# First stage of a fused mLSTM and MLP kernel: u spread by TensorE, decays by a product, weights split in quarters on GpSimd

## The chip, the cores and the metric

The kernel runs on 1 core of one Trainium2 chip. The metric is device time in microseconds (us). The engines are PE (TensorE), DVE (VectorE), ACT (ScalarE), POOL (GpSimd) and SP (SyncE, which only issues DMAs here).

## What is computed

An mLSTM recurrence over 4 batches x 8 heads x 768 steps with head size 40, and then two MLP layers over the 3072 tokens of 320 features. Cut from the reference:

```python
for t in range(S):
    m_new = np.maximum(f_gate[:, :, t] + m, i_gate[:, :, t])
    f_stab = np.exp(f_gate[:, :, t] + m - m_new)
    i_stab = np.exp(i_gate[:, :, t] - m_new)
    m = m_new
    C = f_stab[:, :, None, None] * C + i_stab[:, :, None, None] * np.einsum('bhd,bhe->bhde', vt, kt)
    n = f_stab[:, :, None] * n + i_stab[:, :, None] * kt
    h_tilde = np.einsum('bhde,bhe->bhd', C, qt)
    denom = np.maximum(np.abs(np.einsum('bhd,bhd->bh', n, qt)[:, :, None]), 1.0)
    y[:, :, t] = o * h_tilde / denom
...
h = x @ w_in                                   # 320 -> 2048
x = (np.maximum(h, 0) + alpha * np.minimum(h, 0)) @ w_out
h = np.maximum(np.maximum(x @ w1, x @ w2), x @ w3)   # 320 -> 768, three times
out = h @ w_out2
```

## The kernel before

The recurrence is computed in 24 chunks of 128 steps (8 heads at once): within a chunk as masked products, between chunks by a carried state. The chunks are grouped in 7 blocks (of 2, 3, 3, 4, 4, 4 and 4). While the first MLP layer of block b runs on PE, the chunks of block b+1 are computed between its matmuls; the second MLP layer comes last. So only the chunks 0 and 1 (block 0) stand ahead of all matmuls of the MLP. This is the first stage, and its order is `PLAN_FIRST`, written by hand; `block_plan` gives the order after it. Each engine goes through the same list of steps (`EVERY`) and takes out its own part, strictly in order; semaphores join them.

The stages of the first stage, with the lines of before:

- Gates (DVE, L864 to L875): a running maximum over 768 steps for the 32 rows (batch, head), then for each half of the sequence the decay, its sum within a chunk (`U`, by a scan of 128 steps for each chunk, L873) and `V`. `gates_done` counts the halves. The inputs of these instructions are all in SBUF. ACT makes `E` and `W` out of them (L725 to L730), PE transposes `V`, `E`, `W` (L521), and DVE copies the result into `tables` (L883).
- Mask and exponent of a chunk: `U` is stored to DRAM (L413), and each chunk's row is loaded again into all 128 partitions (`load_u`, L408, into `u_bcast`). POOL masks it ("prepare", L1098) and weighs the values with a table (L1091); ACT takes exp with a table as bias ("gate", L769). DVE multiplies the product of queries and keys (PE, L553) with it ("scores", L908).
- The state ("carry"): PE L561 and L568, DVE L920 to L930. Its last step on DVE, L930, adds the decayed state, which POOL makes (`state_decayed`, L1137) from a table of decays. That table is one row of `tables`, stored to DRAM (L439) and loaded into all partitions (L442).
- "values" (PE L583, DVE L940), "finish" (DVE L950 to L961) and "turn" (PE L602, ACT L759, DVE L967 and L968) end a chunk in `x_split`, which the MLP reads. Chunks from the third on also need "pack": the values split in three bf16 parts by ACT (L750, L753) and POOL (L1122, L1125), and the probabilities split by DVE (L912) and POOL (L1131).
- The weights of the first MLP layer are split into a high part (ACT `high_piece`, L707, L711, L712) and the rest (`low_piece`, L365, L369, L371) on DVE or POOL. `PIECES` lists the ten pieces: six of 128 x 1024 for w_in, four of 128 x 1280 for w_out. `ACT_PIECES`, `DVE_PIECES` and `POOL_PIECES` say after which step of the list an engine does which. PE's "hidden" (L627) and "project" (L641 to L646) of block 0 wait for them.

## Time and profile before

| | us |
|---|---|
| median of 3 runs | 793.49 (793.34 to 794.3) |
| the profiled execution | 794.83 |
| its span in the trace | 793.1 |
| PE busy | 745.3 (94%) |
| DVE busy | 477.2 (60%) |
| ACT busy | 310.1 (39%) |
| POOL busy | 184.1 (23%) |

The span is the time from the first to the last instruction in the trace; 1.7 us lie around it. Busy shares are means over the whole span; PE's first 71 us are far less filled than the rest.

### The profile page before, as it was taken

How to read it: one execution, taken by the hardware profiler on the slowest of the kernel's cores; microseconds unless marked ns; L12 is line 12 of the kernel's file. 1: busy time of each engine (PE TensorE's matmuls, PEld its weight loads, DVE VectorE, ACT ScalarE, POOL GpSimd, SP SyncE). 2: the span in 40 equal slices, each digit the busy share in tenths (PEclk: the TensorE clock that was granted, in tenths of full speed). 3: DMA queues.
4: the chain of work that ended last, by engine and by line, in shares of the span. 5: the costliest groups of instructions: out<-in, count | busy, mean ns of one | idle time of the engine just before them, and what ended most of it. 6: DMA issues, size and time to landing. Idle time of an engine off the chain costs nothing.

```text
span 793.1 us, 11547 instructions
## 1 busy us (share of the span) xinstructions
PE 745.3 (94%) x4410; PEld 656.1 (83%) x4410; DVE 477.2 (60%) x823; ACT 310.1 (39%) x648; POOL 184.1 (23%) x187
## 2 busy tenths in 40 slices
PE   2556999999999999999999999999999999999997
PEld 2545999999998888888888888888888888888886
DVE  6345888878978786888688754934242432434222
ACT  4354455455356444644554245431211212121211
POOL 4277533334524332434233200000000000000000
PEclk9757999999999999999999999999999999999999
DMA  7961232223223221231110053030110202000000
GB/s 203 259 215 61 78 102 72 101 75 105 69 81 105 88 79 58 87 105 61 42 54 1 1 182 120 1 110 4 36 39 0 74 1 74 0 34 1 34 0 34
DMA packets 40057, 56.37 MB, mean 71 GB/s; under 512 B 3457, under 2 KB 29058, under 8 KB 39618
## 3 DMA queue, kind: packets, MB, share of 16 engines
q1 hardware_dynamic: 39570, 54.57, 22.3%
q10 hardware_dynamic: 432, 1.06, 0.4%
q8 instruction: 35, 0.57, 0.3%
q14 instruction: 20, 0.16, 0.1%
HBM read 47.65 MB, written 7.96 MB: 70 GB/s over the span
## 4 chain that ended last, share of the span: by engine, by line
PE 83%; DVE 7%; POOL 3%; DMA 2%; SPq 2%; issue 1%; ACT 1%; ACTq 0%; DVEq 0%; POOLq 0%
PE bank L663 25%; PE bank L627 20%; PE bank L641 5%; PE bank L643 5%; PE bank L642 5%; PE bank L553 4%; PE bank L677 3%; PE bank L679 3%; PE bank L678 3%; PE bank L645 3%; PE bank L646 2%; PE bank L561 1%; PE bank L568 1%; POOL wproj L369 1%; PE bank L590 1%
## 5 line engine op out<-in xcount | busy, mean ns | idle before, releaser
L627 PE MATMUL bank<-x_split,w_hi 128*128 128x512 f32 (+2 forms) x560 | 170.7, 372 | 2.2 <-ACT x_split L759 2.2
L627 PE MATMUL bank<-x_split,w_lo 128*128 128x512 f32 (+2 forms) x336 | 121.9, 365 | 0.0
L627 PEld LDWEIGHTS bank<-x_split,w_hi 128*128 128x128 f32 x560 | 103.9, 191 | 16.2 <-ACT x_split L759 2.6
L795 ACT ACTIVATE g_full<-bank 128x512 f32<-128x512 f32 (+2 forms) x112 | 59.8, 534 | 143.7 <-PE bank L627 142.0
L993 DVE SCALAR_TENSOR_TENSOR g_full<-g_full,beta,bank 128x512 f32<-128x512 f32 (+2 forms) x112 | 74.7, 667 | 38.4 <-ACT g_full L795 37.5
L641 PE MATMUL bank<-g_hi,wproj 128*128 128x512 f32 (+2 forms) x224 | 84.9, 379 | 3.5 <-DVE g_lo L974 3.5
L1014 DVE TENSOR_TENSOR best<-bank,first_of_max 128x512 f32<-128x512 f32 x36 | 24.9, 692 | 103.9 <-PE bank L663 77.4
L804 ACT ACTIVATE g_hi<-g_full 128x512 fp32r<-128x512 f32 (+2 forms) x112 | 63.2, 564 | 61.4 <-DVE g_full L993 61.3
L974 DVE TENSOR_TENSOR g_lo<-g_full,g_hi 128x512 fp32r<-128x512 f32 (+2 forms) x112 | 70.3, 627 | 18.9 <-ACT g_hi L804 18.1
L643 PE MATMUL bank<-g_hi,wproj 128*128 128x512 f32 (+2 forms) x224 | 81.5, 364 | 0.0
L642 PE MATMUL bank<-g_lo,wproj 128*128 128x512 f32 (+2 forms) x224 | 81.4, 363 | 0.0
L834 ACT ACTIVATE g_hi<-best 128x512 fp32r<-128x512 f32 x36 | 22.8, 632 | 130.4 <-DVE best L1018 130.4
L663 PE MATMUL bank<-x_split_b,w_hi 128*128 128x512 f32 x270 | 71.5, 394 | 0.0
L1131 POOL TENSOR_TENSOR prob<-prob_rest 128x512 bf16<-128x512 f32 x44 | 49.1, 1117 | 93.8 <-DVE prob_rest L912 93.8
L627 PEld LDWEIGHTS bank<-x_split,w_lo 128*128 128x128 f32 x336 | 64.4, 192 | 7.4
L663 PE MATMUL bank<-x_split_a,w_hi 128*128 128x512 f32 x270 | 70.3, 390 | 0.0
L769 ACT ACTIVATE u_bcast<-u_bcast,tables 128x128 f32<-128x128 f32 x192 | 59.8, 390 | 9.1 <-POOL u_bcast L1098 9.1
L663 PEld LDWEIGHTS bank<-x_split_b,w_hi 128*128 128x128 f32 x270 | 50.0, 188 | 10.4
L663 PEld LDWEIGHTS bank<-x_split_a,w_hi 128*128 128x128 f32 x270 | 50.0, 188 | 9.5
L553 PE MATMUL bank<-q_t,k_t 120*128 120x128 f32 x384 | 51.3, 290 | 4.5 <-DVE inner L940 4.5
L553 PEld LDWEIGHTS bank<-q_t,k_t 120*128 120x128 f32 x384 | 50.3, 206 | 5.8 <-DVE inner L940 4.6
L641 PEld LDWEIGHTS bank<-g_hi,wproj 128*128 128x128 f32 x224 | 42.5, 190 | 9.0 <-issue 2.8
(115 smaller groups left out, 1399.6 us busy)
## 6 DMA issues: line engine op xcount, KB each, us to landing
u_bcast<-u_scratch SPq DMA_DIRECT2D x24, 512.0 KB, 4.4
kv<-in_kv SPq DMA_DIRECT2D x24, 324.0 KB, 3.0
out<-final SPq DMA_DIRECT2D x6, 640.0 KB, 3.8
q_t<-in_q_t SPq DMA_DIRECT2D x24, 120.0 KB
k_t<-in_k_t SPq DMA_DIRECT2D x48, 60.0 KB
wproj_raw<-in_w_out SPq DMA_DIRECT2D x4, 640.0 KB, 10.5
o_gate<-in_o_gate SPq DMA_DIRECT2D x4, 640.0 KB, 4.8
w_raw<-in_w_max SPq DMA_DIRECT2D x2, 1152.0 KB, 6.5
```

The costliest lines, as they stand in the source:

```text
L553: ins = pe.matmul(ps[:, k * L:(k + 1) * L], kt[0:KR, c, h, :], qt[0:KR, c, h // KH, :], start=True, stop=True)
L627: ins = pe.matmul(ps[:, 0:cols], w[:, a, f], xs[:, x, 0:cols], start=(m == 0), stop=(m == 7))
L641: pe.matmul(acc[a][:, 0:cols], wa, hi, start=(j == 0), stop=False)
L642: pe.matmul(acc[a][:, 0:cols], wa, lo, start=False, stop=False)
L643: pe.matmul(acc[a][:, 0:cols], wl, hi, start=False, stop=(j == J1 - 1))
L663: ins = pe.matmul(ps[:, :], w[:, a, cols], x2[b2 % 2][:, x, :], start=(k == 0), stop=(k == 7))
L769: ins = act.activation(ub[:, c, h, :], ub[:, c, h, :], ACT.Exp, bias=tables[:, 0, ch, h:h + 1])
L795: act.activation(gf[:, n % GF_SLOTS, 0:cols], hid[j % HID_BANKS][:, 0:cols], ACT.Relu, scale=-1.0).then_inc(neg_done, 1)
L804: act.activation(gh[:, n % G_SLOTS, 0:cols], gf[:, n % GF_SLOTS, 0:cols], ACT.Copy).then_inc(g_hi_done, 1)
L974: dve.tensor_tensor(gl[:, n % G_SLOTS, 0:cols], gf[:, n % GF_SLOTS, 0:cols], gh[:, n % G_SLOTS, 0:cols].bitcast(F32), ALU.subtract).then_i ...
L993: dve.scalar_tensor_tensor(out=g, in0=g, scalar=beta[:, j:j + 1], in1=hid[j % HID_BANKS][:, 0:cols], op0=ALU.mult, op1=ALU.add).then_inc(h ...
L1131: pool.tensor_tensor(prob_3[:, heads, :], prob_r[:, heads, :], high(prob_r[:, heads, :]), ALU.subtract).then_inc(prob_split, 1)
```

## The change

Only the first stage and the weight pieces change.

1. For the chunks 0 and 1 (`ON_PE` = 2) `u` is not stored and loaded again. PE spreads it: for each half of the heads 4 matmuls of bf16 that put the mask into a bank (`later`, MASKED where a key is later), and 4 f32 matmuls that add the head's row of `U` (`bcast`). POOL doesn't mask these chunks, and ACT reads the bank.
2. The table of decays is a product of PE with a matrix that has ones in its last row (`decays`), copied by DVE; the store and the load are gone.
3. The gates are computed in the spans of chunks 0 to 1 and 2 to 5 instead of two halves; `chain` 0, 1 and 2 stand at three places of the list. Chunk 0 has no "carry" product, since the state ahead of it is zero.
4. w_in is loaded and split in four quarters (12 pieces of 128 x 512); w_out stays in four. POOL does all rests, DVE none.
5. The clears of `k_t` are on DVE, one for each slot; `i_gate` is loaded by ACT's queue. On SP's queue `o_gate` of block 0 comes after chunk 0. The store and the load of `u` for chunk 2 are issued by ACT ("exps" 1), which waits for the store between the two.
6. The turn of chunk 0 stands ahead of the finish of chunk 1, and the exponents of chunk 2 ("gate" 2) behind both turns; the high parts of w_out's last two quarters stand on ACT among the first "hidden" steps.

```diff
-    steps = [("prepare", 0), ("prepare", 1), ("gate", 0, 0), ("gate", 0, 1), ("scores", 0), ("carry", 0),
-             ("gate", 1, 0), ("gate", 1, 1), ("values", 0), ("scores", 1), ("finish", 0, 0), ("finish", 0, 1),
-             ("prepare", 2), ("carry", 1), ("values", 1), ("gate", 2, 0), ("gate", 2, 1), ("pack", 2, 0),
-             ("finish", 1, 0), ("finish", 1, 1), ("pack", 2, 1), ("prepare", 3)]
-    return steps + [("turn", 0), ("turn", 1)]
+    return [("chain", 0), ("exps", 0), ("products", 0), ("turns", 0), ("bcast", 0), ("turns", 1), ("bcast", 1),
+            ("tables", 0), ("gate", 0, 0), ("gate", 0, 1), ("chain", 1), ("tables", 1), ("prepare", 0),
+            ("scores", 0), ("chain", 2), ("values", 0), ("carry", 0), ("gate", 1, 0), ("gate", 1, 1),
+            ("exps", 1), ("prepare", 1), ("products", 1), ("scores", 1), ("finish", 0, 0), ("finish", 0, 1),
+            ("turns", 2), ("tables", 2), ("decays",), ("carry", 1), ("values", 1), ("turn", 0), ("finish", 1, 0),
+            ("finish", 1, 1), ("turn", 1), ("prepare", 2), ("gate", 2, 0), ("gate", 2, 1),
+            ("pack", 2, 0), ("pack", 2, 1), ("prepare", 3)]
...
-
-PIECES = [("in", a, half) for half in range(2) for a in range(3)] + [("out", n, 0) for n in range(4)]
-ACT_PIECES = {("gate", 0, 1): (2, 3), ("gate", 1, 1): (3, 5), ("gate", 2, 1): (5, 6), ("pack", 2, 1): (6, 10)}
-DVE_PIECES = {("carry", 0): (2, 3)}
-POOL_PIECES = {("prepare", 2): (3, 5), ("prepare", 3): (5, 10)}
+TASKS = [(part, s[1]) for s in EVERY for part in parts_of(s)]
+
+IN_PARTS, OUT_PARTS = 4, 4
+
+
+def pieces():
+
+    order = [("in", a, 0) for a in range(3)]
+    for q in range(1, IN_PARTS):
+        order += [("in", a, q) for a in range(3)] + [("out", q - 1, 0)]
+    return order + [("out", OUT_PARTS - 1, 0)]
+
+
+PIECES = pieces()
+IN_END = [PIECES.index(("in", 2, q)) + 1 for q in range(IN_PARTS)]
+OUT_END = [PIECES.index(("out", n, 0)) + 1 for n in range(OUT_PARTS)]
+
+ACT_PIECES = {("start",): (0, 3), ("gate", 0, 1): (3, 6), ("exps", 1): (6, 10), ("gate", 2, 1): (10, 14),
+              ("hidden", 0, 1): (14, 15), ("hidden", 0, 2): (15, 16)}
+POOL_PIECES = {("start",): (0, 3), ("prepare", 0): (3, 6), ("prepare", 1): (6, 10), ("prepare", 2): (10, 11),
+               ("pack", 2, 1): (11, 14), ("scores", 2): (14, 15), ("carry", 2): (15, 16)}
+
+LOAD_U_AFTER = ("exps", 1)
...
-            load_o(0)
-            sp.wait_ge(cleared, 1)
-            load_chunk(0)
-
-            sp.wait_ge(gates_done, 1)
-            store_u(slice(0, CPH), 0, u_stored[0])
-            sp.wait_ge(u_stored[0], 16)
-            load_u(0)
-            sp.wait_ge(cleared, 2)
-            load_chunk(1)
-            load_u(1)
-            load_w1(sp, 0, (2,))
-
-            sp.wait_ge(tables_set, 2)
-            sp.dma_start(decay_d, tables[L - 1:L, 1, :, :].rearrange("p c h -> p (c h)")).then_inc(decay_stored, 16)
-            load_w1(sp, 1, range(3))
-            sp.wait_ge(decay_stored, 16)
-            sp.dma_start(tables[:, 3, :, :].rearrange("p c h -> p (c h)"), decay_d.to_broadcast([128, NCH * H])
-                         ).then_inc(decay_loaded, 16)
-            load_chunk(2)
-            load_u(2)
-
-            sp.wait_ge(gates_done, 2)
-            store_u(slice(CPH, CPS), 0, u_stored[1])
...
+            sp.wait_ge(q_cleared, 1)
+            sp.wait_ge(k_cleared, 1)
+            load_chunk(0)
+            load_o(0)
+            sp.wait_ge(k_cleared, 2)
+            load_chunk(1)
+            load_w1(sp, 1, range(3))
+            sp.wait_ge(k_cleared, 3)
+            load_chunk(2)
+            load_out(0)
+            load_w1(sp, 2, range(3))
+
+            sp.wait_ge(gates_done, 2)
+            for b in range(1, B):
+                store_u(sp, 0, b, u_stored[1])
+            load_w1(sp, 3, range(3))
+            load_out(1)
+            load_chunk(3)
+            sp.wait_ge(u_stored[0], 16)
+            load_u(sp, 3)
+            load_out(2)
+            load_out(3)
             load_o(1)
-            sp.wait_ge(u_stored[1], B * 16)
-            for ch in range(SLOTS, NCH):
+            sp.wait_ge(u_stored[1], (B - 1) * 16)
...
+            def bcast(ch):
+
+                if ch == 0:
+                    pe.wait_ge(pick_set, 1)
+                    pe.wait_ge(later_set, 2)
+                    pe.wait_ge(gates_done, 1)
+                t = slice(ch * L, (ch + 1) * L)
+                for g in range(NG):
+                    ps = spread[ch][g]
+                    for k in range(HG):
+                        pe.matmul(ps[:, k * L:(k + 1) * L], ident_b[:, :], later[:, :], start=(k == 0), stop=False,
+                                  skip_group_check=True)
+                    for k in range(HG):
+                        ins = pe.matmul(ps[:, k * L:(k + 1) * L], pick[:, g * HG + k, :], gates[0:B * H, U, t],
+                                        start=False, stop=True, skip_group_check=True)
+                    ins.then_inc(spread_out, 1)
+
+            def decays():
+
+                pe.wait_ge(last_set, 1)
+                pe.wait_ge(tables_set, 3)
+                pe.matmul(acc[0][:, 256:256 + NCH * H], last[:, :], tables[:, 1, :, :].rearrange("p c h -> p (c h)"),
+                          start=True, stop=True).then_inc(decays_out, 1)
...
-                        pe.wait_ge(w_split_dve, 3)
-                    if b == 0 and j == J1 // 2:
-                        pe.wait_ge(w_split, 3)
+                        pe.wait_ge(tables_set, 4)
+                    if b == 0 and not j % (J1 // IN_PARTS):
+                        pe.wait_ge(w_split, IN_END[j * IN_PARTS // J1])
...
+            def exps(p):
+
+                first, end = SPANS[p]
+                act.wait_ge(gates_done, p + 1)
+                if p:
+                    store_u(act, ON_PE, 0, u_stored[0])
+                t = slice(max(first, 1) * L, end * L)
+                act.activation(gates[0:B * H, E, t], gates[0:B * H, U, t], ACT.Exp)
+                for c in range(first, end):
                     t = slice(c * L, (c + 1) * L)
                     ins = act.activation(gates[0:B * H, W, t], gates[0:B * H, V, t], ACT.Exp,
                                          bias=gates[0:B * H, U, (c + 1) * L - 1:(c + 1) * L])
                 ins.then_inc(exps_done, 1)
-                if not half:
...
+                    if ch < ON_PE:
+                        act.wait_ge(spread_out, NG * ch + step[2] + 1)
+                    else:
+                        act.wait_ge(masked, ch - ON_PE + 1)
...
+                if s == LOAD_U_AFTER:
+                    act.wait_ge(u_stored[0], 16)
+                    load_u(act, ON_PE)
...
+            def chain(p):
+
+                first, end = SPANS[1 if p else 0]
+                t, at = slice(first * L, end * L), max(first * L, 1)
+                now, before = slice(at, end * L), slice(at - 1, end * L - 1)
+                if p < 2:
+                    if p == 0:
+                        dve.wait_ge(gates_loaded, 32)
+                    start = M_START if p == 0 else g[M_RUN][:, first * L - 1:first * L]
+                    link(dve.tensor_tensor_scan(g[M_RUN][:, t], g[F_RAW][:, t], g[I_RAW][:, t], start, ALU.add, ALU.max))
+                    dve.tensor_tensor(g[F_RAW][:, now], g[F_RAW][:, now], g[M_RUN][:, before], ALU.add)
+                    link(dve.tensor_tensor(g[I_RAW][:, t], g[I_RAW][:, t], g[M_RUN][:, t], ALU.subtract))
+                    link(dve.tensor_tensor(g[DECAY][:, now], g[F_RAW][:, now], g[M_RUN][:, now], ALU.subtract))
+                if p != 1:
+                    for c in range(first, end):
+                        tc = slice(c * L, (c + 1) * L)
+                        ins = dve.tensor_tensor_scan(g[U][:, tc], g[ONES][:, tc], g[DECAY][:, tc], 0.0, ALU.mult, ALU.add)
+                    link(ins)
+                    dve.tensor_tensor(g[V][:, t], g[I_RAW][:, t], g[U][:, t], ALU.subtract).then_inc(gates_done, 1)
...
+                dve.wait_ge(decays_out, 1)
+                dve.tensor_copy(tables[:, 3, :, :].rearrange("p c h -> p (c h)"), acc[0][:, 256:256 + NCH * H]
+                                ).then_inc(tables_set, 1)
+                dve.wait_ge(alpha_loaded, 16)
+                dve.tensor_scalar(beta[:, :], alpha_sb[:, :], -1.0, 1.0, ALU.mult, ALU.add)
 
...
                 if kind == "prepare":
-                    pool.wait_ge(u_loaded[c], 16 * nth)
-                    mask(ch)
+                    if ch >= ON_PE:
+                        pool.wait_ge(u_loaded[c], 16 * ((ch - ON_PE) // SLOTS + 1))
+                        mask(ch)
                     if ch == 0:
-                        pool.wait_ge(tables_set, 1)
-                    if ch == CPH:
                         pool.wait_ge(tables_set, 2)
+                    if ch == ON_PE:
+                        pool.wait_ge(tables_set, 3)
                     pool.wait_ge(nat_loaded[c], 16 * nth)
...
+            for n in range(*POOL_PIECES[("start",)]):
+                low_piece(pool, n, w_split)
             for s in PLAN_FIRST:
```

Where the rows of POOL stand, from the third chunk's preparation in the program of before (w_lo and wproj are the weight pieces, prob_69 is the third part of the probabilities):

```order
L1098 AFFINE_SELECT u_bcast<-u_bcast 128x1024 [waits u_loaded2]
L1091 TENSOR_TENSOR v_weighted<-kv,tables 128x328 [waits kv_loaded2]
L365 TENSOR_TENSOR w_lo<-w_raw,w_hi 128x1024 [waits weights_high] x2
L1137 TENSOR_TENSOR state_decayed<-state,tables 120x328 [waits state_ready,decay_loaded]
L1122 TENSOR_TENSOR v_rest<-kv,v_parts 128x320 [waits v_hi]
L1125 TENSOR_TENSOR v_parts<-v_rest,v_parts 128x8x40 [waits v_mid]
L1098 AFFINE_SELECT u_bcast<-u_bcast 128x1024 [waits u_loaded0]
```

And in the changed program, from the second chunk's preparation to the same place:

```order
L1220 TENSOR_TENSOR v_weighted<-kv,tables 128x328 [waits kv_loaded1]
L406 TENSOR_TENSOR wproj<-wproj_raw,wproj 128x4x256 [waits weights_high]
L408 TENSOR_TENSOR wproj<-wproj_raw,wproj 128x4x64
L402 TENSOR_TENSOR w_lo<-w_raw,w_hi 128x512 [waits weights_high] x3
L1270 TENSOR_TENSOR state_decayed<-state,tables 120x328 [waits state_ready,tables_set]
L1227 AFFINE_SELECT u_bcast<-u_bcast 128x1024 [waits u_loaded2]
L1220 TENSOR_TENSOR v_weighted<-kv,tables 128x328 [waits kv_loaded2,tables_set]
L406 TENSOR_TENSOR wproj<-wproj_raw,wproj 128x4x256 [waits weights_high]
L408 TENSOR_TENSOR wproj<-wproj_raw,wproj 128x4x64
L1255 TENSOR_TENSOR v_rest<-kv,v_parts 128x320 [waits v_hi]
L1258 TENSOR_TENSOR v_parts<-v_rest,v_parts 128x8x40 [waits v_mid]
L402 TENSOR_TENSOR w_lo<-w_raw,w_hi 128x512 [waits weights_high] x3
```

Ahead of the state's decay stand two half pieces of w_in before, and now a piece of w_out and three quarter pieces; a piece of w_out stands ahead of `v_rest`.

POOL further on in the changed program, from the fourth chunk's preparation to the decay for the third chunk and what follows it:

```order
L1227 AFFINE_SELECT u_bcast<-u_bcast 128x1024 [waits u_loaded0]
L1220 TENSOR_TENSOR v_weighted<-kv,tables 128x328 [waits state_out,kv_loaded0]
L1264 TENSOR_TENSOR prob_69<-prob_rest 128x512 [waits prob_rest] x2
L406 TENSOR_TENSOR wproj<-wproj_raw,wproj 128x4x256 [waits weights_high]
L408 TENSOR_TENSOR wproj<-wproj_raw,wproj 128x4x64
L1270 TENSOR_TENSOR state_decayed<-state,tables 120x328 [waits state_ready]
L406 TENSOR_TENSOR wproj<-wproj_raw,wproj 128x4x256 [waits weights_high]
L408 TENSOR_TENSOR wproj<-wproj_raw,wproj 128x4x64
```

Before, one piece of w_in and all four of w_out stood between the preparation and the two splits of probabilities, and nothing on either side of the decay; now two pieces of w_out stand around the decay.

## Rows read from the trace of the kernel before

**Rows 1.** Busy time by stretch: us, PE, PEld, DVE, ACT, POOL, clock, DMA, GB/s.
```profile
51.00:71.00 20.00, 12.44 (x85) 11.73 (x86) 9.94 (x14) 6.74 (x13) 19.56 (x14) 0.67 0.14 47
```

**Rows 2.** Timeline of PE: start us, us, line, operation, [idle before, releaser].
```profile
48.02 0.87 PE L602 MATMUL bank<-ident,y 128*128 128x128 f32 x3 [1.95 <-DVE y L961]
...
69.02 0.26 PE L590 MATMUL bank<-v_parts,prob 128*128 128x123 bf16 x1 [5.70 <-POOL prob L1131]
...
72.69 0.41 PE L641 MATMUL bank<-g_hi,wproj 128*128 128x256 f32 x1
```

**Rows 3.** Timeline of POOL, same columns.
```profile
3.44 1.80 POOL L1079 MEMSET k_t<- 128x2048 f32 x1
...
36.93 1.09 POOL L1098 TENSOR_SCALAR_AFFINE_SELECT u_bcast<-u_bcast 128x1024 f32<-128x1024 f32 x1 [12.40 <-DMA u_bcast<-u_scratch]
...
38.68 4.65 POOL L365 TENSOR_TENSOR w_lo<-w_raw,w_hi 128x1024 fp32r<-128x1024 f32 x2
43.29 0.73 POOL L1137 TENSOR_TENSOR state_decayed<-state,tables 120x328 f32<-120x328 f32 x1
43.99 0.77 POOL L1122 TENSOR_TENSOR v_rest<-kv,v_parts 128x320 f32<-128x320 f32 x1
...
58.20 2.38 POOL L369 TENSOR_TENSOR wproj<-wproj_raw,wproj 128x1024 fp32r<-128x1024 f32 x1
...
67.16 0.72 POOL L371 TENSOR_TENSOR wproj<-wproj_raw,wproj 128x256 fp32r<-128x256 f32 x1
67.84 2.03 POOL L1131 TENSOR_TENSOR prob<-prob_rest 128x512 bf16<-128x512 f32 x2
```

**Rows 4.** Timeline of DVE: two-input instructions with POOL busy, the last without.
```profile
44.13 0.98 DVE L930 TENSOR_TENSOR state<-state_new,state_decayed 120x328 f32<-120x328 f32 x1 [10.08 <-POOL state_decayed L1137]
...
58.28 2.85 DVE L912 TENSOR_TENSOR prob_rest<-prob 128x512 f32<-128x512 f32 x1
...
70.67 0.50 DVE L930 TENSOR_TENSOR state<-state_new,state_decayed 120x328 f32<-120x328 f32 x1 [7.39 <-POOL state_decayed L1137]
```

**Rows 5.** Timeline of ACT.
```profile
8.17 0.74 ACT L719 ACTIVATE o_gate<-o_gate 128x640 f32<-128x640 f32 x1 [4.63 <-DMA o_gate<-in_o_gate]
...
11.09 0.97 ACT L730 ACTIVATE gates<-gates 32x128 f32<-32x128 f32 x3
11.96 1.99 ACT L707 ACTIVATE w_hi<-w_raw 128x1024 fp32r<-128x1024 f32 x2
...
38.06 2.44 ACT L769 ACTIVATE u_bcast<-u_bcast,tables 128x128 f32<-128x128 f32 x8 [6.57 <-POOL u_bcast L1098]
...
45.17 1.04 ACT L711 ACTIVATE wproj<-wproj_raw 128x1024 fp32r<-128x1024 f32 x1
...
50.17 0.84 ACT L759 ACTIVATE x_split<-bank 128x384 fp32r<-128x384 f32 x2
```

**Rows 6.** Timeline of DVE in the gates and the finish of a chunk.
```profile
5.70 1.75 DVE L864 TENSOR_TENSOR_SCAN gates<-gates 32x768 f32<-32x768 f32 x1 [3.65 <-DMA gates<-in_i_gate]
...
8.53 0.55 DVE L870 TENSOR_TENSOR gates<-gates 32x383 f32<-32x383 f32 x1
9.11 1.04 DVE L873 TENSOR_TENSOR_SCAN gates<-gates 32x128 f32<-32x128 f32 x3
...
20.37 0.69 DVE L908 TENSOR_TENSOR prob<-bank,u_bcast 128x512 f32<-128x512 f32 x1 [0.45 <-ACT u_bcast L769]
```

**Rows 7.** Timeline of PE: the query-key products of two chunks.
```profile
16.49 3.59 PE L553 MATMUL bank<-q_t,k_t 120*128 120x128 f32 x16
...
78.19 1.95 PE L553 MATMUL bank<-q_t,k_t 120*128 120x128 f32 x16
```

**Rows 8.** The chain that ended last, around the table of decays: start us, us.
```profile
17.27 5.87 DMA decay_scratch<-tables
```

**Rows 9.** DMA issues up to 70 us: KB each, median us to landing.
```profile
o_gate<-in_o_gate SPq DMA_DIRECT2D x1, 320.0 KB, 6.4
...
gates<-in_f_gate SPq DMA_DIRECT2D x1, 96.0 KB, 2.6
```

270 lines of the change are left out of this document (155 added, 115 removed).

## The prediction

> **What bounds the kernel now.** I first read the busy time by stretch. From 71 us on PE is filled and nothing of the change lies there, so I take that part as fixed. The stretch from 51 to 71 us is the one to look at: POOL is busy 19.56 of 20 us and PE only 12.44 [rows 1]. PE's timeline names the wait: the values of chunk 2 begin at 69.02, after 5.70 us idle, released by POOL's split of the probabilities [rows 2]. POOL's timeline shows what stood ahead of that split: w_in and w_out pieces without a gap, 2.38 us for 128x1024 and 0.72 for 128x256 [rows 3]. Further back POOL waited 12.40 us for u of chunk 2, masked it at 36.93, did two pieces in 4.65, and only then the decay at 43.29 [rows 3], for which DVE had waited 10.08 [rows 4]. So the early part is a chain of loads, then POOL. PE's first projection after that, of the second hidden tile, starts at 72.69 [rows 2]; I compare with this event, because PE runs on from there.
>
> **The change, step by step.** The times are from the start of the span, and where an operation has another width I scale the row.
>
> *Until the second `gates_done`.* A clear of one k_t slot takes 0.9 (half of 1.80) [rows 3]; behind DVE's clears SP issues chunk 0's queries and keys from about 3.4, an estimate. They land between 8.5 and 12.4 (2.6 and 6.4 behind an issue that ends at about 6) [rows 9]; I take 9.0, since little else is under way. PE is in order: the products of chunk 0, 3.59 at the slow pace [rows 7], stand ahead of the transposes of V, so DVE gets the first table at 13.3. ACT waits for `o_gate`, now issued at about 6.2: landing 8.8 to 12.6 by the same rows, taken as 10.0. From there, by rows 5: sigmoid 0.74, three quarters of w_in at 0.55 (1.99/4 and a little), table load and exponents 2.3 (from the end of the sigmoid, 8.91, to 12.06 it is 3.15, with a wait and a wider first exponent in it), gates of chunk 0 2.44, three quarters, gates of chunk 1: 21.2.
> DVE's chain 1 (512 columns): scan 1.2, three operations at 0.7 [rows 6], so 3.3 without hindrance: 16.6. But the first three quarter pieces now run on POOL, 1.2 each (half of 2.34) [rows 3]. The rows say what that costs: with POOL busy L912 took 2.85, and L930 0.98 where it takes 0.50 [rows 4]; it started at 44.13 and ended at 45.11, 0.35 behind the end of POOL's 43.99 + 0.77 [rows 3]. I add two waits of 0.65: 17.9. Tables 0.4, scores of chunk 0 2 x 0.69 [rows 6]: 19.7. Chain 2 is four scans of 0.35 and one operation of 0.7: 21.8 if nothing hinders it. Beside it POOL has three pieces and one weighing, 3.6 us. If each DVE instruction lets one of POOL's through, chain 2 ends at 25.4. The trace has no scan beside a reading POOL, and no two such DVE instructions in a row; its bounds are 21.8 and 25.4, and I take the middle, 23.6.
>
> *Until both chunks are turned.* ACT: store of u 0.3, exponents of 512 columns 0.7 and four of 0.32 [rows 5]: 25.9. It then waits for the store (issued by 23.9, 2.6 to land [rows 9]: 26.5), issues the load 0.4, and makes w_out's first high piece (1280 columns at 1.04 for 1024, 1.3 to 1.4 [rows 5]): 28.3. DVE does the values and the state of chunk 0 meanwhile, and PE the products of chunk 1 in 1.95, warm [rows 7]; with its scores behind them DVE reaches the finish of chunk 0 at 26.9, and needs about 1.9. Its last operations meet POOL's 2.38 us instruction, which begins at 28.3. Nothing or all of it, so 1.2: 30.0. Tables, decay product and its copy: 32.0. This is 3 us before POOL wants it, so the product in place of the store (5.87 [rows 8]) and load comes off the path. POOL is late next: w_out piece 2.38 + 0.72, three quarters at 1.25, decay 0.73 [rows 3], 35.9. Then it goes straight on to the mask of chunk 2, 1.09, and DVE's state step stands behind it, as behind `v_rest` at 43.99: 37.4. From the state step's end to PE's turn it was 2.9 before (45.11 to 48.02 [rows 2, 4]). The turn of chunk 0 now stands in between: 0.87 on PE, 0.42 on ACT [rows 5] and some 0.7 on DVE, of which 0.56 lie beside the values. With the second turn's 0.87 and 0.42 that is 5.6: ACT has x_split of chunk 1 at 43.0, against 51.01 before (50.17 + 0.84 [rows 5]). Eight us are gained here.
>
> *The tail.* Here the change gives back. Gates of chunk 2 2.44 and the high piece 1.4 now stand behind the turns: 46.9. POOL's w_out piece 3.1 (it waits for that high piece), `v_rest` 0.77, ACT 0.48, third part 0.78: 52.0. Three quarters of w_in 3.75, with three DVE instructions of about 0.4 let through: 57.0. Mask 1.09 and weighing 0.73: 58.8, then 2.03 for the splits [rows 3]. PE begins the values at 59.8, 9.2 before the 69.02 of now. But the next w_out piece (3.1) now stands ahead of the decay (0.73): 64.6, and another one right behind it. DVE's state step loses its turn to that one's 2.38, the same pattern as at 44.13 [rows 4], and then 0.35: 67.3. One more POOL instruction of 0.6 and the rest of g, 0.3: the projection starts at 68.2. Before it started 1.5 after the state step's end (70.67 + 0.50 [rows 4]) with PE filled ahead of it. Now PE stands idle for some 4 us ahead of it and comes back at the slow pace (3.59 against 1.95 for the same products [rows 7]); the projection and one hidden tile at 0.8 more each, less what before had slow too, cost 0.8. 72.69 - 68.2 - 0.8 = 3.7 us gained.
>
> What costs nothing: the mask and spread matmuls. A chunk has eight f32 products of the size in rows 7 and eight bf16 ones, which I put at a quarter of those (an estimate, f32 showing in two records each): 2.4 us warm, 4.5 slow. Chunk 0's lie from 13.0 on, beside ACT's loads and exponents up to 14.7; chunk 1's are wanted at 18.8, and at the slow pace would come at 23. That would cost nothing still, as ACT's next step waits for chain 2 until 23.6. The quarter loads cost nothing either: the last is issued at 23.6 and wanted after 43.
>
> The sum goes against the profiled execution, 794.83: 791.1. The median of the runs is 1.34 lower, so 789.8 for it.
>
> **Rivals.**
> *The scans take no turns.* Chain 2 ends 1.8 earlier and chunk 0's finish is over before the w_out piece (1.2): the projection starts 3.0 earlier, gain 6.7, 786.8. For it: no row shows a scan hindered. Against: a scan reads two operands from SBUF, as L930 does, which was.
> *Strict turns.* Chain 2 ends 1.8 later, PE has then been idle over 3 us and makes chunk 1's second group of products at the slow pace (+0.8), and the finish of chunk 0 stands wholly behind the w_out piece (+1.2). 3.8 lost, gain -0.1: 793.6. For it: 2.85 and 0.98 are full waits, not shared bandwidth [rows 4]. The Trainium skill says so outright (SBUF — State Buffer, Who interferes with whom): a DVE instruction with two SBUF inputs contends with a GpSimd one that reads SBUF, under an exclusive lock; the scans would fall under it, and the time by that rule is this rival's. By that rule, L912 and L930 of the trace agree; for scans no row here shows it.
> *Slower: the store of u at the head of ACT's queue.* ACT waits for it and holds the weight pieces, and so POOL. I price it 2.6; the 0.8 KB store of the decays took 5.87 among the weight loads [rows 8]. At 5.87 the gain of 3.7 falls to about 0.4; from 7.5 on the change is slower by over 0.2%, and at 10, as behind a full queue, 789.8 + 7.4 = 797.2. For it: w_in's last quarter and w_out's second are issued in the same microseconds. Against: ACT's own queue holds nothing else by then.
>
> **How the numbers follow.** A run tells some 0.2% (1.6 us) from no change. Chances: my forecast (788.2 to 791.9) 0.38; scans free (785 to 788) 0.24; strict turns (792 to 795) 0.24, a fifth of it still faster; the store 0.14, three quarters of it clearly slower, and some of the strict case slower by a late `o_gate` (2.6 more). Faster 0.38 + 0.24 + 0.04 = 0.66, same 0.19, slower 0.15. The likeliest is 789.8; the range of 8 in 10 goes from 785 to 796.
>
> **What would show it.** First table on DVE near 13.3 and the second `gates_done` near 23.6 (21.8 or 25.4 decide between the rivals); scans of over 0.35 us beside POOL's pieces; ACT's wait for the store of u near 0.6; POOL's first w_out piece at 28.3 and its decay at 35.9; x_split of chunk 1 at 43.0; the values of chunk 2 at 59.8 but the projection of the second tile only at 68.2, with DVE's state step over 2 us long. Wrong would be a DMA that lands late enough to order the early part, queries at 12 or `o_gate` at 12.6, or a PE that waits again behind 75 us.

## The result and the profile after

The changed kernel takes 796.69 us in the median of 5 runs (795.82 to 798.43), the kernel before 793.92 beside it (793.34 to 794.3): a ratio of 1.0035, with a 95% interval of 1.0023 to 1.0047. It is slower by 2.8 us, a little more than these measurements can tell from no change. The two profiled executions, which the traces show, differ by 1.2 us only. The forecast was 789.8, with 785 to 796 as its range. The profiled execution took 795.99, with a span of 794.2 us (before: 794.83 and 793.1).

First the stretch of [rows 1], in the same columns, of the changed kernel. ("Half clock" and "slow pace" below are the lower of PE's two levels, 1.2 against 2.4 GHz, seen in the granted clock or in the durations. "Low parts" are the rests of the weight pieces.)

```profile
51.00:71.00 20.00, 12.49 (x85) 11.34 (x83) 7.63 (x10) 12.85 (x24) 17.88 (x15) 0.71 0.17 54
```

POOL is busy 17.88 us where it was 19.56, and PE 12.49 where it was 12.44. The picture is the old one although everything ahead of it was rewritten. PE's timeline, to be read beside [rows 2]:

```profile
8.73 3.78 PE L631 MATMUL bank<-q_t,k_t 120*128 120x128 f32 x16 [8.73 <-DMA k_t<-in_k_t]
...
20.78 0.61 PE L580 MATMUL bank<-later_keys,ident_bf 128*128 128x128 bf16 x4
21.32 2.07 PE L583 MATMUL bank<-gates,pick_head 32*128 32x128 f32 x8
23.32 3.64 PE L662 MATMUL bank<-kv,prob 128*128 128x41 f32 x16
26.76 1.61 PE L647 MATMUL bank<-v_weighted,kv 128*120 128x128 f32 x6
28.16 3.62 PE L631 MATMUL bank<-q_t,k_t 120*128 120x128 f32 x16
...
47.48 0.87 PE L681 MATMUL bank<-ident,y 128*128 128x128 f32 x3 [3.36 <-DVE y L1083]
...
65.36 0.26 PE L669 MATMUL bank<-v_parts,prob 128*128 128x123 bf16 x1 [0.61 <-POOL prob L1264]
...
73.49 0.58 PE L718 MATMUL bank<-g_hi,wproj 128*128 128x256 f32 x1 [4.26 <-DVE g_lo L1096]
```

The values of chunk 2 (L669) begin 3.7 us earlier than before, at 65.36. The projection of the second tile (L718) begins 0.8 later, after 4.26 us in which PE stands, where it had stood 5.70 ahead of the values. DVE's timeline, with the rows that answer to [rows 4] and to the gates of [rows 6], and three of the finish of chunk 0:

```profile
14.34 1.57 DVE L972 TENSOR_TENSOR gates<-gates 32x512 f32<-32x512 f32 x1
15.84 1.74 DVE L973 TENSOR_TENSOR gates<-gates 32x512 f32<-32x512 f32 x1
17.61 1.64 DVE L974 TENSOR_TENSOR gates<-gates 32x512 f32<-32x512 f32 x1
...
20.75 4.70 DVE L978 TENSOR_TENSOR_SCAN gates<-gates 32x128 f32<-32x128 f32 x4
25.49 0.68 DVE L980 TENSOR_TENSOR gates<-gates 32x512 f32<-32x512 f32 x1
...
33.03 1.18 DVE L1073 SCALAR_TENSOR_TENSOR norm<-inner,norm 128x8 f32<-128x8 f32 x1
...
34.49 1.27 DVE L1077 TENSOR_TENSOR scale<-o_gate,norm 128x320 f32<-128x320 f32 x1
35.80 1.44 DVE L1081 TENSOR_TENSOR y<-inner,scale 128x320 f32<-128x320 f32 x1
...
70.02 2.55 DVE L1050 TENSOR_TENSOR state<-state_new,state_decayed 120x328 f32<-120x328 f32 x1 [6.17 <-POOL state_decayed L1270]
```

And POOL's, to be read beside [rows 3]:

```profile
20.41 3.96 POOL L402 TENSOR_TENSOR w_lo<-w_raw,w_hi 128x512 fp32r<-128x512 f32 x3
...
52.54 2.38 POOL L406 TENSOR_TENSOR wproj<-wproj_raw,wproj 128x1024 fp32r<-128x1024 f32 x1 [10.38 <-ACT wproj L790]
...
57.64 4.64 POOL L402 TENSOR_TENSOR w_lo<-w_raw,w_hi 128x512 fp32r<-128x512 f32 x3
62.24 1.28 POOL L1227 TENSOR_SCALAR_AFFINE_SELECT u_bcast<-u_bcast 128x1024 f32<-128x1024 f32 x1
...
66.17 2.36 POOL L406 TENSOR_TENSOR wproj<-wproj_raw,wproj 128x1024 fp32r<-128x1024 f32 x1
68.49 0.73 POOL L408 TENSOR_TENSOR wproj<-wproj_raw,wproj 128x256 fp32r<-128x256 f32 x1
69.18 0.74 POOL L1270 TENSOR_TENSOR state_decayed<-state,tables 120x328 f32<-120x328 f32 x1
69.87 2.34 POOL L406 TENSOR_TENSOR wproj<-wproj_raw,wproj 128x1024 fp32r<-128x1024 f32 x1
```

Read these as one chain. POOL stands idle for 10.38 us up to 52.54, since ACT makes the high part that it needs only behind the turns and the gates of chunk 2. Then it makes up for this while the attention of chunk 2 waits: the mask of chunk 3 comes at 62.24 and the splits of chunk 2's probabilities only behind it, a w_out piece stands ahead of the decay, and the next one ahead of DVE's state step, which is 2.55 us long where it is 0.50 alone. From there on little differs: from the projection of the second tile to the end of the profiled execution it was 722.1 us before and is 722.5 now.

### The profile page after: what moved, and what is told of

Its sections match the earlier page's. It is cut to its first block, busy times and chain, and to the rows that moved or that the text cites. A ratio compares the mean times of both kernels' runs of the same rounds, so it can differ in the third digit from the quotient of the medians.

```text
span 794.2 us, 11666 instructions
## 1 busy us (share of the span) xinstructions
PE 758.8 (96%) x4454; PEld 668.1 (84%) x4454; DVE 486.8 (61%) x825; ACT 310.0 (39%) x654; POOL 194.3 (24%) x199
## 4 chain that ended last, share of the span: by engine, by line
PE 86%; DVE 7%; POOL 3%; issue 2%; ACT 2%; DMA 0%; SPq 0%; ACTq 0%; DVEq 0%; POOLq 0%
PE bank L740 25%; PE bank L706 20%; PE bank L718 5%; PE bank L720 5%; PE bank L719 5%; PE bank L631 5%; PE bank L754 3%; PE bank L756 3%; PE bank L755 3%; PE bank L723 3%; PE bank L722 3%; PE bank L647 2%; PE bank L639 2%; PE bank L669 1%; DVE g_lo L1096 1%
## 5 line engine op out<-in xcount | busy, mean ns | idle before, releaser
L718 PE MATMUL bank<-g_hi,wproj 128*128 128x512 f32 (+2 forms) x224 | 85.4, 381 | 8.0 <-DVE g_lo L1096 8.0
L857 ACT ACTIVATE u_bcast<-u_bcast,tables 128x128 f32<-128x128 f32 x176 | 54.9, 390 | 0.1
L718 PEld LDWEIGHTS bank<-g_hi,wproj 128*128 128x128 f32 x224 | 42.7, 191 | 13.8 <-DVE g_lo L1096 6.0
```

Of the source, the lines that this page charges most:

```text
L718: pe.matmul(acc[a][:, 0:cols], wa, hi, start=(j == 0), stop=False)
L857: ins = act.activation(ub[:, c, h, :], src, ACT.Exp, bias=tables[:, 0, ch, h:h + 1])
```

## The experiments

The ratios are to the kernel before, run on the same chip, with their 95% intervals; the changed kernel has 1.0035 (1.0023 to 1.0047). The kernel before differs by up to 1.2 us from chip to chip (792.74 to 793.92), so where the text gives what one kernel is worth against another, it is the difference of their ratios times 793.5 us.

| kernel | median us | ratio |
|---|---|---|
| e1: pieces 14, 15 behind the state step | 797.34 | 1.0050 (1.0038 to 1.0063) |
| e2: warm start of PE | 795.68 | 1.0035 (1.0022 to 1.0047) |
| e3: POOL held for the second gates | 797.62 | 1.0050 (1.0036 to 1.0064) |
| e4: u of chunks 0, 1 through DRAM | 799.13 | 1.0083 (1.0069 to 1.0096) |
| e5: pieces 10 to 13 early | 792.46 | 0.9990 (0.9981 to 0.9999) |
| e6: pieces 10 to 15 early | 790.51 | 0.9969 (0.9960 to 0.9979) |
| e7: e6 and warm start | 789.23 | 0.9958 (0.9945 to 0.9971) |
| e8: e7 and POOL held | 788.62 | 0.9948 (0.9935 to 0.9960) |
| e9: e8 and a wait for the rows of chunk 1 | 786.56 | 0.9911 (0.9895 to 0.9928) |
| e10: the kernel before, pieces early | 788.49 | 0.9944 (0.9929 to 0.9959) |
| e11: e6, u through DRAM | 792.91 | 0.9996 (0.9988 to 1.0005) |
| e12: e6, decays through DRAM | 795.82 | 1.0033 (1.0021 to 1.0045) |
| e13: e10 and a wait for the rows of chunk 1 | 790.43 | 0.9964 (0.9953 to 0.9976) |
| e14: e6 and that wait | 788.66 | 0.9949 (0.9934 to 0.9963) |
| e15: e9, turn of chunk 0 later | 786.09 | 0.9916 (0.9901 to 0.9932) |
| e16: changed kernel, PE kept busy | 794.98 | 1.0028 (1.0018 to 1.0038) |
| e17: e15, PE kept busy | 783.93 | 0.9878 (0.9858 to 0.9898) |

### One suspect at a time in the changed kernel: e1 to e4

e1 moves the last two w_out pieces on POOL behind DVE's state step of chunk 2:

```diff
-               ("pack", 2, 1): (11, 14), ("scores", 2): (14, 15), ("carry", 2): (15, 16)}
+               ("pack", 2, 1): (11, 14), ("carry", 2): (14, 16)}
+                        if s == ("carry", 2):
+                            pool.wait_ge(state_ready, 4)
```

> The changed kernel, with one edit: on POOL the third and fourth piece of w_out come behind the state step of chunk 2 (POOL waits for DVE's addition first), not one ahead of the decay and one right behind it. In the trace of the changed kernel the decay for chunk 2 starts at 69.18, DVE's state step takes 2.55 (70.02 to 72.57) and the projection of the second tile starts at 73.49. Theory A (the tail costs what the trace shows): decay at 66.2, state step of 0.5 at 67.0, the projection at 68.3, so 5 us less, 791.7 against 796.7. Theory B (the time is lost earlier and the pieces only take each other's place): the pieces then stand ahead of POOL's work for chunk 3, PE waits there, and the gain is under 2 us.

The state step is free now, 0.50 long at 68.23. But PE waits again, at 77.83:

```profile
77.83 0.58 PE L718 MATMUL bank<-g_hi,wproj 128*128 128x256 f32 x1 [3.58 <-DVE g_lo L1096]
```

DVE's timeline of e1 says for what. Between 68.81 and 75.4 POOL does the two pieces, and a `norm` operation on 128x8 elements takes 2.23 us; g_lo is queued behind it:

```profile
72.60 2.23 DVE L1072 TENSOR_SCALAR norm<-inner 128x8 f32<-128x8 f32 x1
```

So the wait moved from the state step to the finish, and nothing was gained (1.2 us slower than the changed kernel, with intervals that overlap).

e2 puts twelve products of the identity, whose results nobody reads, ahead of everything on PE; e3 holds POOL until the second `gates_done` before it takes the second quarter of w_in:

```diff
+            for n in range(12):
+                pe.matmul(acc[1][:, 0:128], ident[:, :], ident[:, :], start=True, stop=True)
```
```diff
+                if s == ("prepare", 0):
+                    pool.wait_ge(gates_done, 2)
```

> The changed kernel, with 12 products of the identity with itself (f32, 128x128) on PE ahead of everything, into a bank that is not yet used; they add nothing to the result. PE was at the slow pace from 8.73 to 31.8 in the changed kernel's trace, although it was hardly ever idle. Theory A (PE's pace is a bound of the early part): if the extra work raises the pace, chunk 1's products end near 29 instead of 31.8, and x_split of chunk 1 comes 2 to 3 us before 48.88: 794. Theory B (DVE against POOL sets the early part): same time within 1 us even where the pace is raised. A third outcome is that the pace does not stay up over the products with 32 rows, and then nothing changes and A stays open.

> The changed kernel, with POOL held before its pieces of the second quarter of w_in until the second gates_done, so that DVE's chain 2 has the SBUF for itself. In the changed kernel its four scans took 4.70 us together where four at 0.35 are 1.4. Theory B (turns between DVE and POOL set the early part): scans 1.4, the second gates_done near 22.5 instead of 26.2, and 1 to 3 us less at the end. Theory A (PE's pace bounds the early part up to 31.8): the scans shrink as in B, but chunk 1's products still end near 31.8 and the time is the same within 1 us.

In e2 the first products take 2.19 instead of 3.78, but PE stands 2.29 ahead of the transposes of E and W, and the spread of chunk 1 is at 2.07 for half the heads as before, where chunk 0 had 1.15. The projection is 1.9 earlier, at 71.61, but the ratio is that of the changed kernel. The rows behind the projection say where most of it went. From there to its next wait PE does the same instructions, in 17.4 us in the changed kernel (73.49 to 90.91) and in 18.7 in e2 (71.61 to 90.33): by the durations the half clock lasts 2.9 us there and 5.7 here. So 0.6 us of the 1.9 is left. In e3, from 74.03 to 92.92, it is 18.9. How long the half clock lasts behind the last long wait is thus a term of over 1 us that no edit set, and differences of that size between two traces prove little.

In e3 the four scans take 1.35 together, so this is what turns with POOL cost them:

```profile
21.13 1.35 DVE L978 TENSOR_TENSOR_SCAN gates<-gates 32x128 f32<-32x128 f32 x4
22.51 0.68 DVE L980 TENSOR_TENSOR gates<-gates 32x512 f32<-32x512 f32 x1
```

The second gates are ready at 23.2 instead of 26.2, and nothing of the three arrives at the finish of chunk 0: DVE stands 2.47 until PE has the values of chunk 0, and the products of chunk 1 end at 32.2 instead of 31.8, as late as the first products were. PE's queue is the bound there, and the gates only behind it. The finish itself ends 1.0 us earlier (36.45), but then PE's values of chunk 1 take 3.48 instead of 2.24, and that is lost too.

e4 sends u of chunks 0 and 1 through DRAM again, with POOL's mask, and leaves the spread out.

> The changed kernel with one part undone: u of the chunks 0 and 1 goes through DRAM and POOL's mask again, as before the change, and PE spreads nothing. The rest of the change stays. Theory A (PE's pace and load bound the early part): PE loses some 10 us of work ahead of chunk 0's values, chunk 1's products end by 29, and the time falls by 2 to 3 us to about 794. Theory B (DVE against POOL): two masks of 1.1 more on POOL, one of them ahead of chain 2, and the time rises by 1 to 2 us. If the spread is what wins something, as the change means it to, the time rises by 2 or more.

It costs 3.8 us over the changed kernel. The spread is worth something, even at the slow pace.

### The place of the low parts: e5, e6, e10

ACT is idle from 31.4 to 44.2 in the changed kernel and POOL from 42.2 to 52.5. e5 and e6 let ACT round the last pieces there, and POOL follow. e6 is

```diff
-ACT_PIECES = {... ("exps", 1): (6, 10), ("gate", 2, 1): (10, 14),
-              ("hidden", 0, 1): (14, 15), ("hidden", 0, 2): (15, 16)}
+ACT_PIECES = {... ("exps", 1): (6, 14), ("turn", 0): (14, 16)}
-POOL_PIECES = {... ("prepare", 2): (10, 11),
-               ("pack", 2, 1): (11, 14), ("scores", 2): (14, 15), ("carry", 2): (15, 16)}
+POOL_PIECES = {... ("prepare", 2): (10, 16)}
```

and e5 the same with pieces 14 and 15 left where they were.

> ScalarE rounds pieces 10 to 13 (the second w_out quarter and the last w_in quarter) right behind the exponentials of the second span, where it stood idle from 31.4 to 44.2, and GpSimd takes their low parts from 42 on, where it stood idle for 10.4 us, instead of from 52.5 to 62.2; the rest is the changed kernel. Theory A (the lead was lost because 7.7 us of these low parts stand on GpSimd between the turns and the attention of chunk 2): weights of chunk 2 masked by 55 instead of 62.2, state decayed by 65 or before instead of 69.9, second project step at 69 to 71 instead of 73.5, time 792 to 795. Theory B (VectorE and GpSimd share the port, so the low parts cost VectorE what they spare later): products of chunk 2 earlier, but the x_split and finish operations of VectorE longer by as much, second project step not before 73, time 796 to 798.

> As the kernel with pieces 10 to 13 early, and also both last w_out quarters: their low parts (6.5 us) run on GpSimd between 42 and 57 and none is left between the scores of chunk 2 and its state step. Theory A (low parts in that stretch are the loss): state step of chunk 2 ends by 64 instead of 72.6, second project step bound by TensorE at 67 to 70, time 790 to 794. Theory B (14 us in a row on GpSimd hold back v_rest of chunk 2 and finish 1 on VectorE): values of chunk 2 not before 65, second project step at 72 or later, time 795 to 798.

e5 is 3.6 us faster than the changed kernel and e6 5.2: no other single edit comes near. The waits of PE in e6 between 45 and 80 us, by its timeline:

```profile
54.88 0.87 PE L679 MATMUL bank<-ident,y 128*128 128x128 f32 x3 [9.27 <-DVE y L1081]
56.33 0.58 PE L704 MATMUL bank<-x_split,w_hi 128*128 128x256 f32 x1 [0.58 <-ACT x_split L840]
65.41 0.36 PE L716 MATMUL bank<-g_hi,wproj 128*128 128x256 f32 x1 [1.00 <-DVE g_lo L1094]
...
72.85 0.39 PE L716 MATMUL bank<-g_hi,wproj 128*128 128x256 f32 x1 [0.47 <-DVE g_lo L1094]
```

The turn of chunk 1 is 7.4 us later than in the changed kernel (54.88 against 47.48), since the finish of chunk 1 now lies beside 13 us of low parts; the values of chunk 2 are not earlier. Yet the kernel is 5.2 faster. The row at 72.85 is the projection of the fourth tile, where the changed kernel begins the second at 73.49: from 60 to 77 us PE is busy 15.53 us against 10.07, at a granted clock of 0.99 against 0.62. One late start costs less than three waits with the half clock after each: from 45 to 80 us PE stands 13.1 us in the changed kernel and 11.3 in e6, so less than half of the 5.2 is waiting, and the rest is pace. This is read from two traces, and no run varies the clock alone. Theory A had the projection of the second tile (68.42) and the time right; theory B the late values, which did not decide.

e10 takes the kernel before and changes a single table entry:

```diff
-POOL_PIECES = {("prepare", 2): (3, 5), ("prepare", 3): (5, 10)}
+POOL_PIECES = {("prepare", 2): (3, 5), ("pack", 2, 1): (5, 10)}
```

> The kernel before, with one table entry changed: the low parts of pieces 5 to 9 (16.4 us of GpSimd) stand behind the second part of pack of chunk 2, at 46, instead of behind the preparation of chunk 3, at 52.4. GpSimd stood idle from 46.1 to 50.7 there. Theory A (the place of the low parts sets the end of the first stage in either kernel): values of chunk 2 at 63.5 to 65.5 instead of 69.0, time 789.5 to 791.5, so most of what the early order gained is to be had without the new first stage. Theory B (finish of chunk 1 on VectorE beside them gives it back): turn of chunk 1 at 50 instead of 48, time 792 to 794.

788.49 us, faster than theory A had it, although the turn of chunk 1 moved from 48.02 to 52.78, further than theory B had it (50). This one entry is worth 4.4 us, more than the whole first stage was forecast to be.

### What the parts are worth where the tail is clean: e7, e8, e11, e12

e7 adds the edit of e2 to e6, e8 those of e2 and e3, and e11 that of e4. e12 takes the product with the last row out and sends the decays through DRAM again, stored when the third tables are set.

> All low parts early and 12 products of the identity ahead of everything on TensorE. If the slow clock of TensorE between 8.7 and 31.8 costs its own share beside the place of the low parts, the gain of 1 us in the median of the warm kernel adds to that of the early low parts: 1 to 2 us below the kernel with all early. If one bound hides the other, the same as that kernel within 0.5.

> As the last one, and GpSimd held until the gates of the second span are done, so that the four scans run alone. With a warm TensorE the second span should be worth something now, if TensorE's pace had hidden it: products of chunk 1 at 25 instead of 28 and the time 1 to 3 us below the last kernel. If TensorE falls back to 1.2 GHz in the pause ahead of the turns, as it did at 16.4 to 26, no gain beyond 0.5.

> The changed kernel with all low parts early (790.5), and u of chunks 0 and 1 broadcast through DRAM again instead of spread by TensorE. With the last low parts out of the way the 2.4 us that the same step cost in the changed kernel should be seen again or grow, if the spread is worth something by itself: 792.5 to 795. If GpSimd's row of low parts bounds now and the attention of chunks 0 and 1 does not, within 0.5 of 790.5.

> The changed kernel with all low parts early (790.5), and the decays sent through DRAM again, stored once the last tables are set, instead of by a product with the last row. In the kernel before the load took 5.87 us at 17.3, hidden; here it starts at about 39. State_decayed of chunk 1 at 44 to 46 instead of 39.5, everything behind it on GpSimd (mask, low parts) 4 to 6 later, time 792 to 796. If the wait is hidden by the 9.3 us for which TensorE waits for the turn of chunk 1, within 0.5 of 790.5.

The spread is worth 2.1 us here. The decay product is worth 5.1, as POOL's timeline of e12 shows:

```profile
48.17 0.73 POOL L1270 TENSOR_TENSOR state_decayed<-state,tables 120x328 f32<-120x328 f32 x1 [10.73 <-DMA tables<-decay_scratch]
```

It says what the round trip costs in this order of work, where the last tables come at 38. Before, it cost something too: the store lay at 17.27, on the chain that ended last [rows 8], and SP issued the load of u for chunk 2, for which POOL waited 12.40 [rows 3], only behind it. What the product would be worth in the kernel before was not tried. The warm start and the hold give 0.9 and 0.8, each less than can be told here, and 1.7 together, where the intervals just meet.

### The finish of chunk 1 beside POOL: e9, e13, e14, e15

e9 makes POOL wait, ahead of piece 13, until the rows of chunk 1 are written; e14 does it without the warm start and the hold of e3; e13 does it in the kernel before, ahead of piece 5; e15 puts the turn of chunk 0 behind the finish of chunk 1 in e9's plan.

```diff
+                    if n == 13:
+                        pool.wait_ge(y_ready, 2)
```

> All low parts early, warm TensorE and GpSimd held as before, and GpSimd also waits ahead of piece 13 until the output rows of chunk 1 are written. In the kernel without this wait VectorE needs 9 us for them (scale 2.35, y 0.90, the copy 2.21, norm 0.79 and 1.18) beside 14 us of low parts, and TensorE waits 9.28 for the turn of chunk 1 at 53.0. Theory A (shared port): norm, scale, y and copy in about 3 us behind piece 12, turn of chunk 1 at 49 to 51, time 785.5 to 788. Theory B (the first hidden products are not what bounds, chunk 2 on GpSimd is): turn earlier, but second project step not earlier than 71, time within 1 us of that kernel.

> The kernel before with the low parts behind pack of chunk 2 (788.5), and GpSimd waits ahead of them (from 44.4 on) until the rows of chunk 1 are written, which VectorE alone does in 3 us: it starts at 46 instead of 44.4, the turn of chunk 1 moves from 52.8 to 47, the first hidden product from 54.2 to 48.5. Theory A (finish of chunk 1 beside GpSimd costs time in either kernel): 785.5 to 787.5, so the old first stage with the low parts placed well is level with the new one (786.6). Theory B (the mask of chunk 3 and the low parts before it bound, and they start later): 788 to 790, and the new first stage is worth 2 us at its best.

> The changed kernel with all low parts early and the wait ahead of piece 13, without the warm start of TensorE and without the hold of GpSimd for the gates. Those two gave 1.9 us on the kernel without this wait (790.5 to 788.6), and the wait 2.1 on top of them (788.6 to 786.6). If the shares add, 788.4; if the wait works only where chunk 1 is early, 789.5 or more.

> The kernel of 786.6 with the turn of chunk 0 behind the finish of chunk 1 in the plan instead of ahead of it, as it stood in the kernel before. There VectorE waits 0.96 for ScalarE's x_split of chunk 0 at 44.58 and spends 0.71 on its own before it takes up norm of chunk 1. Theory A: norm 1.6 earlier, turn of chunk 1 at 46.4 instead of 48.0, 785.5 to 786.3. Theory B: both turns then stand in a row on TensorE and both x_splits on ScalarE and VectorE, first hidden product not before 49.4, 786.5 to 787.

The same operations of DVE, first in e8 beside POOL's low parts, then in e9, where POOL stops at 46.1:

```profile
45.04 0.79 DVE L1074 TENSOR_SCALAR norm<-inner 128x8 f32<-128x8 f32 x1
45.86 1.18 DVE L1075 SCALAR_TENSOR_TENSOR norm<-inner,norm 128x8 f32<-128x8 f32 x1
47.08 0.20 DVE L1077 RECIPROCAL norm<-norm 128x8 f32<-128x8 f32 x1
47.32 2.35 DVE L1079 TENSOR_TENSOR scale<-o_gate,norm 128x320 f32<-128x320 f32 x1
49.70 0.90 DVE L1083 TENSOR_TENSOR y<-inner,scale 128x320 f32<-128x320 f32 x1
50.63 2.21 DVE L1085 COPY y<-y 128x64 f32<-128x64 f32 x1
```
```profile
45.34 0.78 DVE L1074 TENSOR_SCALAR norm<-inner 128x8 f32<-128x8 f32 x1
46.16 0.17 DVE L1075 SCALAR_TENSOR_TENSOR norm<-inner,norm 128x8 f32<-128x8 f32 x1
46.36 0.20 DVE L1077 RECIPROCAL norm<-norm 128x8 f32<-128x8 f32 x1
46.59 0.49 DVE L1079 TENSOR_TENSOR scale<-o_gate,norm 128x320 f32<-128x320 f32 x1
47.12 0.49 DVE L1083 TENSOR_TENSOR y<-inner,scale 128x320 f32<-128x320 f32 x1
47.64 0.19 DVE L1085 COPY y<-y 128x64 f32<-128x64 f32 x1
```

They take 7.8 us against 2.5, and e9 is 2.9 us faster than e8; e14 is 1.6 faster than e6. The kernel before gains nothing by such a wait (e13 is 1.6 slower than e10, a little beyond theory B). The intervals of these two pairs still touch. There all low parts, 15 us, go behind it, and PE has this row:

```profile
65.22 0.26 PE L590 MATMUL bank<-v_parts,prob 128*128 128x123 bf16 x1 [4.47 <-POOL prob L1131]
```

So with the low parts well placed in either, the new first stage with all three additions is 2.6 us ahead of the old one (e9, e10); with the same placement alone it is 2.0 behind it (e6, e10). The warm start and the early hold were not tried in the kernel before, so the 2.6 is not the worth of the stage alone. e15 and e9 can't be told apart.

### PE kept busy through chunk 1: e16, e17

Eleven more products of the identity stand between the spread of chunk 0 and the transposes of E and W, added to e2 and to e15:

```diff
+                    for m in range(11):
+                        pe.matmul(acc[1][:, 0:128], ident[:, :], ident[:, :], start=True, stop=True)
```

> The changed kernel with the warm start, and 11 more products of the identity between the spread of chunk 0 and the transposes of E and W, where TensorE otherwise stands 2.3 us and falls to 1.2 GHz. If it keeps its clock, spread of chunk 1 takes 3.0 instead of 5.2 us, the values of chunk 0 2.0 instead of 3.6, products of chunk 1 end at 27 to 28 instead of 31.8. Theory A (TensorE's slow pace on chunk 1 is the step by which the prediction failed): finish of chunk 0 starts at 28 or before, x_split of chunk 1 at 44 to 46 instead of 48.9, time 793 to 795. Theory B (chain 2 beside GpSimd, done at 26.2, holds the exponentials and the weights as long anyway): finish 0 at 28 to 29 but x_split of chunk 1 not before 47, time as with the warm start alone, 795.7 within 0.7.

> The fastest kernel so far (786.1) with the 11 products as well. There GpSimd is held, so chain 2 is done at 23; TensorE at full pace would give the products of chunk 1 by 26 and finish 0 by 26.5 instead of 31. Theory A: turn of chunk 1 2 to 3 us before 45.8, 783.5 to 785. Theory B (weights on GpSimd, held until the gates and then 14 us long, set the rest): 785.5 to 786.5.

PE's timeline of e16 has the spread and the values of chunk 0 at full pace, and then the next bound:

```profile
20.06 1.15 PE L589 MATMUL bank<-gates,pick_head 32*128 32x128 f32 x8
21.14 1.98 PE L668 MATMUL bank<-kv,prob 128*128 128x41 f32 x16
22.95 0.90 PE L653 MATMUL bank<-v_weighted,kv 128*120 128x128 f32 x6
25.76 3.76 PE L637 MATMUL bank<-q_t,k_t 120*128 120x128 f32 x16 [1.91 <-DVE inner L1066]
```

PE waits 1.91 for a copy of DVE that stands behind the four scans (4.69 in this kernel), and the products of chunk 1 are slow again. The finish of chunk 0 starts 2.3 us earlier than in the changed kernel, at 30.16, but needs 6.2 us beside POOL instead of 5.0; the turn of chunk 1 comes 1.0 earlier. Neither theory fits whole: the finish of chunk 0 starts later than both had it, x_split of chunk 1 ends at 47.9, which theory B allows, and 794.98 lies just inside theory A's range and just outside theory B's. By the ratios it is 0.6 better than the changed kernel, less than can be told.

e17 is the fastest kernel of the study, 783.93, and 3.0 faster than e15 (2.2 by the medians, 1.5 between the two profiled executions). The finish of chunk 0 starts at 28.30 in it against 30.19 in e15, but the decays' copy is at 35.86 against 35.93: the finish takes 5.8 us beside POOL's pieces instead of 4.0. Its time is the one that theory A gave, but not by theory A's way: the turn of chunk 1 is at 46.20, not before e15's 45.83. What differs in the traces is one later wait: e15 stands 2.07 for g_lo at 80.27 and goes on at half the clock, e17 stands 1.38 at 80.59 and keeps it, and is 1.2 us ahead at the next products (82.59 against 83.79). Why the one falls and the other doesn't was not tried.

## Why the prediction was wrong, by its own steps

**The tail was right, only late.** From x_split of chunk 1 on, every step came 5.3 to 5.9 us after its forecast: x_split at 48.88 (forecast 43.0), POOL's three quarters done at 62.28 (57.0), values of chunk 2 at 65.36 (59.8), state step done at 72.57 (67.3) and over 2 us long as forecast, projection at 73.49 (68.2). The lateness was there before the tail began.

**The step that failed** is the one on the products of chunk 1: "in 1.95, warm [...] DVE reaches the finish of chunk 0 at 26.9", with the spread, which "would cost nothing still". The spread of chunk 1 did end at 23, and ACT did wait for chain 2 anyway. But PE works in order, and behind the spread stand the values and the state of chunk 0 and the products of chunk 1: 3.64, 1.61 and 3.62, from 23.32 to 31.78. DVE started the finish at 32.43. The price was looked for on ACT, and it lay in PE's own queue. The forecast granted the slow pace to the spread up to 23 and took the products right behind it as warm. The spread of chunk 1 was also a little longer than its 4.5: 5.15, from 18.24 on.

**Chain 2 and the scans.** The rival of strict turns was right on them: 4.70 us for four scans that take 1.35 alone, second `gates_done` at 26.17, where the rival had 25.4 and the forecast 23.6. Chain 1 ended at 19.25, not 17.9, by the same cause. The Trainium skill (SBUF — State Buffer, Who interferes with whom) says that a DVE instruction with two SBUF inputs contends with a GpSimd one that reads SBUF. The rows agree for scans, 4.70 beside POOL's pieces and 1.35 without them. Alone it was not what bounded: with the scans free (e3) the finish of chunk 0 started no earlier. Together with a faster PE it counts. In e17, with free scans and PE kept busy, the finish starts at 28.30, 4.1 of the 5.5 us that it was late, where e16 alone gives 2.3 and e3 none. (What else differs in e17 lies behind that place.)

**The finish of chunk 0** was put at 1.9 and 1.2 for a wait, and took 5.04 (32.43 to 37.47). Three operations took 1.18, 1.27 and 1.44 instead of 0.17, 0.49 and 0.49, each beside a piece of POOL. This gives back what a faster PE brings (6.2 us in e16, 5.8 in e17). Neither suspect alone moves the projection by over 1.9 of the lost 5.3 us (71.61 in e2, 72.50 in e16, 74.03 in e3), and how much of it belongs to which has no single answer: each hides the other.

**The sum.** The projection 5.3 late of its forecast, less 0.4 because the half clock behind it cost 0.36 instead of 0.8: 4.9 of 6.9. The other 2.0 is the step from the profiled execution to the median, 1.34 down in the forecast and 0.70 up in the measurement.

**The rivals.** The store of u on ACT's queue did not hold ACT: u was stored from 26.20 on and loaded at 28.08, with the exponents between. (The rival's threshold of 7.5 should have been 7.9: 2.6, the gain of 3.7 and the 1.6 of a run.) None of the rivals has the reason why the kernel is slower. The forecast priced what the changed order does with the low parts (64.6 for the decay, 67.3 for the state step), took it as given, and did not ask what another place for them was worth. e6 and e10 show that this is as large as any term, 5.2 and 4.4 us, in a kernel where POOL stands idle for 10 us just ahead of it.

## What to carry to other kernels

When a product is moved to an engine that works in order, price it against what is queued behind it there, at the slow pace of that engine, before looking at who reads its result. Where GpSimd and VectorE both have long work, look first for a stretch where GpSimd stands idle and VectorE has nothing urgent, and put the work there: one table entry gave more than a rewritten stage. And one long wait early can be cheaper than three short ones late, when each is followed by the half clock, as e6 suggests. An event that comes earlier in the trace is a gain only if the clock behind it is the same: of e2's 1.9 us two thirds went to a longer stretch at the half clock.
